# A linear recurrence with two dense layers on one core: transposes a slot sooner, a second tile for the inverse, x awaited in parts

## The reference, cut to what matters

```python
def _attn_ref(r, k, v, w, a, b):            # batch 4, heads 8, 768 tokens, head size 40
    for t in range(S):
        y[:, :, t] = einsum('bhd,bhde->bhe', rt, state)
        Sa = einsum('bhde,bhe->bhd', state, at)
        state_decay = state * wt[:, :, None, :] - einsum('bhd,bhe->bhde', Sa, bt)
        state = state_decay + einsum('bhd,bhe->bhde', vt, kt)
x = y as (3072 tokens, 320)
h = x @ w_in; g = maximum(0.01 * h, h); x = g @ w_out                    # 2048 wide
out = (1 / (1 + exp(-(x @ w_gate))) * (x @ w_val)) @ w_out2              # 1536 wide
```

## Time and profile before

| what | value |
|---|---|
| median of 3 runs | 1114.42 us (1110.23 to 1117.06) |
| profiled execution | 1112.1 us, span 1110.3 us |
| granted TensorE clock, mean | 0.972 |
| TensorE busy | 1046.9 us (94%), 16106 products and as many weight loads |
| VectorE busy | 617.0 us (56%) |
| ScalarE busy | 406.4 us (37%) |
| GpSimd busy | 142.9 us (13%) |
| idle of TensorE before products `a` (L642), ended by GpSimd | 23.3 us in 6 waits |

### The profile page before, as it was taken

One profiled execution on the slowest core, in us unless ns is written; L12 is line 12 of the kernel. 1 busy time (PEld: TensorE's weight loads), 2 busy tenths in 40 slices (PEclk: granted clock), 3 DMA queues, 4 the chain that ended last, 5 costly groups with the idle time before them and its releaser, 6 DMA issues.

```text
span 1110.3 us, 37363 instructions
## 1 busy us (share of the span) xinstructions
PE 1046.9 (94%) x16106; PEld 889.8 (80%) x16106; DVE 617.0 (56%) x2026; ACT 406.4 (37%) x830; POOL 142.9 (13%) x179
## 2 busy tenths in 40 slices
PE   2977979999998999999999999999999999999998
PEld 2866868787887877787887788888888888888887
DVE  7888898869687777776663244343232222323221
ACT  2243334345444443543443345432222232222222
POOL 6313130312213130303000000000000000000000
PEclk9987679999999999999999999999999999999999
DMA  5657254354425343533433043120202002020000
GB/s 173 174 171 187 60 131 95 89 111 108 112 63 134 87 112 64 153 81 73 105 90 63 9 149 115 62 85 1 62 1 63 1 3 59 1 62 1 24 1 24
DMA packets 133863, 87.68 MB, mean 79 GB/s; under 512 B 98274, under 2 KB 113634, under 8 KB 133700
## 3 DMA queue, kind: packets, MB, share of 16 engines
q1 hardware_dynamic: 126740, 62.85, 23.1%
q0 software_dynamic: 6960, 22.45, 6.8%
HBM read 66.39 MB, written 18.87 MB: 77 GB/s over the span
## 4 chain that ended last, share of the span: by engine, by line
PE 88%; issue 4%; DMA 3%; DVE 2%; POOL 2%; SPq 1%; ACT 1%; ACTq 0%; POOLq 0%; DVEq 0%
PE bank L824 17%; PE bank L874 12%; PE pair L874 12%; PE bank L839 4%; PE bank L840 4%; PE bank L841 4%; PE bank L894 4%; PE bank L892 4%; PE bank L893 4%; PE bank L910 2%; PE bank L799 2%; PE bank L843 2%; PE bank L844 2%; PE bank L786 2%; PE bank L642 2%
## 5 line engine op out<-in xcount | busy, mean ns | idle before, releaser
L1330 DVE TENSOR_TENSOR g_lo<-g_full,g_hi 128x512 fp32r<-128x512 f32 x168 | 120.7, 718 | 216.6 <-ACT g_hi L1082 216.4
L1082 ACT CAST g_hi<-g_full 128x512 fp32r<-128x512 f32 x168 | 104.4, 621 | 134.7 <-DVE g_full L1383 131.6
L824 PE MATMUL bank<-x_hi,w_up 128*128 128x512 f32 x480 | 136.6, 415 | 5.3 <-ACT x_hi L1092 3.2
L1278 DVE TENSOR_TENSOR prod<-t_unit,p_unit 128x31 f32<-128x31 f32 (+4 forms) x720 | 131.1, 222 | 5.4 <-ACT t_unit L1016 3.2
L1283 DVE TENSOR_TENSOR t_unit<-t_unit,prod 128x31 f32<-128x31 f32 (+4 forms) x720 | 132.8, 224 | 0.8
L1075 ACT ACTIVATE g_full<-bank 128x512 f32<-128x512 f32 x96 | 57.5, 599 | 188.7 <-PE bank L824 188.6
L824 PEld LDWEIGHTS bank<-x_hi,w_up 128*128 128x128 f32 x480 | 86.6, 192 | 24.8 <-ACT x_hi L1092 3.3
L1383 DVE TENSOR_TENSOR g_full<-pair,h_sb 128x512 f32<-128x512 f32 x36 | 24.9, 692 | 112.7 <-PE pair L874 112.0
L824 PE MATMUL bank<-x_lo,w_up 128*128 128x512 f32 x288 | 82.7, 396 | 0.0
L839 PE MATMUL bank<-g_hi,w_dn 128*128 128x512 f32 x192 | 77.5, 404 | 0.0
L1383 DVE TENSOR_TENSOR g_full<-bank,h_sb 128x512 f32<-128x512 f32 x36 | 24.9, 692 | 94.6 <-PE bank L874 86.3
(11 more groups left out here) (149 smaller groups left out, 2406.4 us busy)
## 6 DMA issues: line engine op xcount, KB each, us to landing
p_unit<-p_dram SPq DMA_DIRECT2D x48, 128.0 KB, 2.9
stage<-in_w_out POOLq DMA_DIRECT2D x7, 640.0 KB, 5.5
v_tok<-in_vT SPq DMA_DIRECT2D x12, 320.0 KB, 3.0
v_nu<-in_vN SPq DMA_DIRECT2D x24, 160.0 KB, 5.9
x<-y_sb SPq DMA_DIRECT2D x48, 80.0 KB
k_sb<-in_kF POOLq DMA_DIRECT2D x22, 160.0 KB, 3.6
v_sb<-in_vF SPq DMA_DIRECT2D x22, 160.0 KB
r_sb<-in_rF SPq DMA_DIRECT2D x22, 160.0 KB
```

Source lines behind the costliest of these rows:

```text
L824: last = nc.tensor.matmul(up_bank(m)[:], lhs, rhs, start=(e == 0), stop=(e == len(products) - 1))
L1082: nc.scalar.copy(g_hi[:, m % 2], g_full[:]).then_inc(g_hi_ready, 1)
L1278: nc.vector.tensor_tensor(terms, t_unit[:, e:m:2, t:t + 1].to_broadcast([P, rows, rest]), p_unit[:, t, t + 1:C].unsqueeze(1).to_broadcast( ...
L1330: nc.vector.tensor_tensor(g_lo[:, m % 2], g_full[:], g_hi[:, m % 2].bitcast(F32), ALU.subtract).then_inc(g_lo_ready, 1)
```

## The change

Seven edits. TensorE's `kb` and ScalarE's copies of them move from slot 7 to slot 6 of each window. `t_unit` gets a second half, taken in turn by units, and `act_t_unit` waits for the store of the unit before the last instead of the last; it stands in slot 7 of every window. `first` writes its eight columns into four, upper and lower partitions side by side, so that the copy to `u_first` is 160 wide instead of 320, and `p_cross` is half as large. The first up group of a block waits for each third of `x_hi` and `x_lo` ahead of the product that reads it. `act_out` waits for each of the four batches by a semaphore of its own. The fill entry ("sn", 0) goes from 56 to 40. `dve` reads and writes `t_unit[:, u % 2]` in all columns. The order of SyncE, GpSimd and VectorE is the same.

```diff
-        p_cross = sb(ctx, "p_cross", [P, 2, 2, TQ, C])
+        p_cross = sb(ctx, "p_cross", [P, 2, 2, TQ // 2, C])
...
-        t_unit = sb(ctx, "t_unit", [P, C // 2, C])
+        t_unit = sb(ctx, "t_unit", [P, 2, C // 2, C])
...
-                    sp.dma_start(dst[z], t_unit[z * MX:(z + 1) * MX]).then_inc(t_stored, 16)
+                    sp.dma_start(dst[z], t_unit[z * MX:(z + 1) * MX, u % 2]).then_inc(t_stored, 16)
...
-                    last = nc.tensor.matmul(o[first_rows(i, q), q * D:(q + 1) * D], t_sb[upper(i), c, q, 0:C],
+                    last = nc.tensor.matmul(o[first_rows(i, q), q % HQ * D:(q % HQ + 1) * D], t_sb[upper(i), c, q, 0:C],
                                             rhs_sb[upper(i), q], start=True, stop=True)
...
-                    last = nc.tensor.matmul(rhs_place(q)[lower(i)], p_cross[first_rows(i, q), u % 2, c, q],
-                                            u_first[first_rows(i, q), q], start=False, stop=True,
+                    last = nc.tensor.matmul(rhs_place(q)[lower(i)], p_cross[first_rows(i, q), u % 2, c, q % HQ],
+                                            u_first[first_rows(i, q), q % HQ], start=False, stop=True,
                                             skip_group_check=True)
...
             blk, f = divmod(m, NF1)
-            if f == 0:
-                pe.wait_ge(x_hi_ready, 3 * (blk + 1))
-                pe.wait_ge(x_lo_ready, 3 * (blk + 1))
...
             for e, (lhs, rhs) in enumerate(products):
+                if f == 0 and e < 3:
+                    pe.wait_ge(x_hi_ready, 3 * blk + e + 1)
+                elif f == 0 and e >= 5:
+                    pe.wait_ge(x_lo_ready, 3 * blk + e - 4)
                 last = nc.tensor.matmul(up_bank(m)[:], lhs, rhs, start=(e == 0), stop=(e == len(products) - 1))
...
                 last = nc.tensor.matmul(o, g_lo[:, par, tok], wt[:, 0, f % GT], start=False, stop=(f == NF2 - 1))
+                if f == NF2 - 1 and b < B - 1:
+                    last.then_inc(out_multiplied, 1)
             last.then_inc(down_multiplied, 1)
...
-        FILL = {("kb", -1): 2, ("sn", 0): 56,
+        FILL = {("kb", -1): 2, ("sn", 0): 40,
...
-                    elif s == 7 and soon:
+                    elif s == 6 and soon:
                         pe_kb(pe, n + 2)
                         pe_kb(pe, n + 3)
                         fill(pe, "kb", g)
...
-                    last = nc.scalar.mul(p_cross[first_rows(i, q), u % 2, c, q:q + HQ],
+                    last = nc.scalar.mul(p_cross[first_rows(i, q), u % 2, c],
                                          src[upper(i), q:q + HQ, C:L], -1.0)
...
-            wait(act, t_stored, 32 * u)
-            if u > 0:
-                columns_done(act, u - 1, C - 1)
-            nc.scalar.copy(t_unit[:].rearrange("p r t -> p (r t)"), restart[:, 1:2].to_broadcast([P, C // 2 * C])
+            wait(act, t_stored, 32 * (u - 1))
+            nc.scalar.copy(t_unit[:, u % 2].rearrange("p r t -> p (r t)"), restart[:, 1:2].to_broadcast([P, C // 2 * C])
                            ).then_inc(zeros_set, 1)
...
-            nc.scalar.copy(u_first[:], bank[bank_of("first", n)][:, 0:DM].rearrange("p (q d) -> p q d", d=D)
+            nc.scalar.copy(u_first[:, 0:HQ], bank[bank_of("first", n)][:, 0:HQ * D].rearrange("p (q d) -> p q d", d=D)
                            ).then_inc(bank_emptied[bank_of("first", n)], 1)
...
-            act.wait_ge(down_multiplied, M1 + NF2 * (blk + 1))
             act.wait_ge(o_stored, 48 * NJ)
             wait(act, o2_stored, 64 * blk)
             for b in range(B):
+                if b < B - 1:
+                    act.wait_ge(out_multiplied, (B - 1) * blk + b + 1)
+                else:
+                    act.wait_ge(down_multiplied, M1 + NF2 * (blk + 1))
                 nc.scalar.copy(o_tok(b), bank[DOWN2[b]][:, 0:DM]).then_inc(o2_evicted, 1)
...
                     elif s == 6 and soon:
                         act_sn(act, n + 2)
-                        if later and g >= 2:
-                            act_t_unit(act, g + 2)
-                    elif s == 7:
-                        if soon:
-                            act_kb(act, n + 2)
-                            act_kb(act, n + 3)
-                        if later and g < 2:
-                            act_t_unit(act, g + 2)
+                        act_kb(act, n + 2)
+                        act_kb(act, n + 3)
+                    elif s == 7 and later:
+                        act_t_unit(act, g + 2)
```

More of the change, by code:

```diff
@@ L190, in rwkv_mlp_kernel @@
         o_stored = sem("o_stored")
+        out_multiplied = sem("out_multiplied")
         o2_evicted = sem("o2_evicted")
@@ L1015, in act_t_unit @@
                 rows = slice(z * MX, (z + 1) * MX)
-                last = nc.scalar.copy(t_unit[rows].rearrange("p r t -> p (r t)")[:, z::C + 2],
+                last = nc.scalar.copy(t_unit[rows, u % 2].rearrange("p r t -> p (r t)")[:, z::C + 2],
                                       restart[rows, 0:1].to_broadcast([MX, C // 2]))
@@ L1277, in inverse_columns @@
                     wait(dve, column_ready[e], done[e])
-                    nc.vector.tensor_tensor(terms, t_unit[:, e:m:2, t:t + 1].to_broadcast([P, rows, rest]),
+                    nc.vector.tensor_tensor(terms, t_unit[:, u % 2, e:m:2, t:t + 1].to_broadcast([P, rows, rest]),
                                             p_unit[:, t, t + 1:C].unsqueeze(1).to_broadcast([P, rows, rest]), ALU.mult
@@ L1282, in inverse_columns @@
                     dve.wait_ge(column_multiplied[e], done[e] + 1)
-                    nc.vector.tensor_tensor(t_unit[:, e:m:2, t + 1:C], t_unit[:, e:m:2, t + 1:C], terms, ALU.add
+                    nc.vector.tensor_tensor(t_unit[:, u % 2, e:m:2, t + 1:C], t_unit[:, u % 2, e:m:2, t + 1:C], terms, ALU.add
                                             ).then_inc(column_ready[e], 1)
```

## The result

The changed kernel took 1141.78 us (median of 4 runs, 1138.70 to 1145.39) beside 1114.43 us (4 runs, 1110.23 to 1117.06) for the kernel before on the same chip: ratio 1.0274, 95% interval 1.0222 to 1.0326. I had forecast 1105.7, with 1 chance in 20 for slower by over 1%. The profiled run of the changed kernel took 1145.39 us and is the slowest of its four; that of the kernel before took 1112.1.

A forecast was written before the change was run, and what follows sets the result against it. TensorE was taken to set the pace from about 160 us, a recurrence's waits before; 1.6 + 1.5 + 3.1 + 1.2 + 1.3 = 8.7 us off the 1114.42 median gave 1105.7 us, range 1098 to 1113.

The forecast's parts named there:

- Transposes a slot sooner: Scan from window 2: k and b transposes 3.7 us sooner, winning 3.1 us of `a_sb` waits and 1.2 of clock.
- Now GpSimd will be through. By TensorE that is worth nothing: Block's `x_lo`: GpSimd's early finish ends the slow casts (4.49 against 1.90 us), worth nothing once x is awaited in parts.
- a stage where it waits for `g_hi` anyway: 0: From window 2, clearing in slot 7 starts VectorE's columns 0 to 6 some 0.5 us later, costing 0.
- My slower one: Early k and b fetch makes x late in five blocks by 3.7 us each, 18.5 lost; near 1124, chance 0.07.
- the unknown of 3 us: Idle times without releaser, some 9 us in eight places between 210 and 630 us, shift: 0, give or take 3.
- The waits for `a_sb` behind 160 us: TensorE's two waits for GpSimd's scaling, 0.81 us at 251.9 and 2.33 at 354.2, were to go: 3.1 us.
- At the fills: Start, fills 56 to 40: 3.6 us idle, clock 0.5, `st` sum at 62 to 63; 1.6 us won.
- Up(0): Block 0's first up group starts 2.0 us sooner with x awaited in parts; `g_lo` of step 0 leaves 0.3.
- start and block 0: Fewer fills were to win 1.6 us at the start, and x part by part 0.3 in block 0.
- The last issue of SyncE: Kernel's end: last copies and issues lie under products, last issue 0.5 us behind the last product; 1.3 us won.
- The second tile: Start: ScalarE's 12.42 us wait and VectorE's 3.25 us delay for the inverse tile go; counted 0, up to 1.0.
- the boundary of code: Start: the 4.07 us idle at 56.45 read as late code; 16 fewer fills move what follows 64 instructions against packets.

The follow-up runs named there:

- e3: Changed kernel with one more wait: from window 3 GpSimd fetches k and b only after slot 0's up group; 1116.15 us, ratio 1.0114.
- e9: Changed kernel with k and b still fetched early, but GpSimd scaling only once VectorE is through column 10; 1110.53 us, ratio 1.0002.
- e7: Changed kernel with the inverse's tile cleared in slot 6 again, from window 2 on; 1134.18 us, ratio 1.0165.
- e10: e9 with slot 0's `g_lo` ahead of columns 7 to 10 and the tile cleared in slot 6; 1110.57 us, ratio 0.9996.
- e12: Kernel before with only VectorE's order in slot 0 changed, `g_lo` ahead of columns 7 to 10; 1113.04 us, ratio 0.9990.
- e2: Kernel before with only the transposes and their copies a slot sooner, the one tile cleared behind them in slot 6; 1132.80 us, ratio 1.0234.
- e11: Changed kernel with slot 0's `g_lo` ahead of columns 7 to 10, the tile cleared in slot 6, no added GpSimd wait; 1110.18 us, ratio 1.0015.
- e5: Changed kernel with k and b fetched early, but GpSimd scaling only after slot 0's `rhs` products, from window 3; 1140.23 us, ratio 1.0220.
- e6: Changed kernel with GpSimd's scaling of a, b and k replaced by memsets from half n = 8 on; 1106.63 us, ratio 0.9976.

## Why the prediction was wrong

**The step that failed** is "Transposes a slot sooner": "GpSimd ... gains the 3.7 us", priced by who waits for GpSimd (`a_sb`, 3.1 us) and not by whom its scaling meets when it runs 3.7 us sooner. The needed rows were in the trace of before: the k scaling at 297.21 against `g_lo` at 296.21 leaves 1.0 us, so 3.7 us sooner must reach into the columns. What the runs showed in place of a gain of 3.1 us is eight waits for `g_lo` of slot 0, 29.0 us, and 13.3 us more of busy time in the scan. The same step also missed that the transposes had been TensorE's cover for this `g_lo`: 3.5 us of slack before, 0.9 left. Without GpSimd's early scaling this costs nearly nothing (2.0 us of waits in e3, 1.5 in e9); with it nearly the whole 4.98 us becomes a wait. I had the mechanism in hand, read from `x_lo` (4.49 against 1.90 us), and carried it only to the place where the collision ends: "Now GpSimd will be through. By TensorE that is worth nothing". It did end: `x_lo` is at 686 ns at the median and at most 693 in the changed kernel. The collision went to the columns, where e9 shows that it is worth some 30 us. The Trainium skill, SBUF — State Buffer, section Who interferes with whom, says that a VectorE instruction with two SBUF inputs and a GpSimd instruction that reads SBUF shut each other out. The columns have two SBUF inputs, and for VectorE the 4.98 us lost beside 4.84 us of four scalings agree with it; GpSimd's own scalings there hardly show it, with 1.18 to 1.28 us.

**The second size missed** is "a stage where it waits for `g_hi` anyway: 0" for the later clearing. It is true of the `g_lo` of slot 7 and not of the next one: with columns 0 to 10 in one stretch, VectorE had 0.9 us of slack at `g_lo` of slot 0 (257.13 against 257.99) in the changed kernel without the collision. e7 puts the place of the clearing at 8 to 12 us of the 27, from 4 runs each and over two batches, so roughly; of waits its trace has 3.9 us less. It costs only because the slack had been used up: in e9 it stands where the change has it, and e10, which moves it, gains nothing.

**The rivals.** My slower one had x late by the early fetch; in the changed kernel's trace TensorE waits 0.72 us for x at 150.39 and nowhere behind it. The right mechanism was none of them, and the range had to miss. The range had a fault of its own: its lower end takes in the unknown of 3 us, its upper end does not, and with it all bounds together would end near 1116.

**What came as forecast.** The waits for `a_sb` behind 160 us, 3.1 us, are gone, but they are back where the scaling is held back (4.1 us in six in e9). At the fills there are 3.69 us idle at 47.40 (3.6 forecast), four records in 1.15 us behind it, the short idle time inside `st` (1.37 at 60.03, in place of 4.07), and the `st` sum at 61.94 (62 to 63 forecast, 64.26 before). But 1.1 of these 2.3 us stood before the first of the fills (36.49 against 37.61), ahead of anything that the fills could have done, so 1.2 us are theirs and the rest is luck. Up(0) starts at 150.39, and `g_lo` of step 0 limits what is kept: 159.11 against 160.62. That is 1.5 us, beside the 1.9 that start and block 0 were to bring, and it is within the scatter: this `g_lo` stands at 154.49 in e12, which has the start of the kernel before, and at 154.8 to 160.9 in the eleven traces with the changed start. So no gain of the start is shown to reach the scan. The v transfer took a part of it (2.58 us at 155.57), which I had not named. The last issue of SyncE is at 1141.34; TensorE's last product ends near 1140.75, so the last issue comes 0.6 us behind it instead of 1.84: 1.25 won, 1.3 forecast. From the dense stage's first `x_lo` to the end of the span it is 401.9 us against 403.0 in the kernel before. The second tile took VectorE's idle time for `t_unit` in the start away and gave nothing, as said.

**Left open.** These terms, without the transposes, make some 3 to 4 us. e9 has them, and its interval leaves room for 4 us of gain at most; it does not show one. Start and scan differ by several us from run to run: the first `x_lo` came at 144.9 us in e12 and at 151.8 in the profile of before, with the same order of work up to there, and I did not find out why. Whether the boundary of code really moved, as I had read the 4.07 us, stays a reading. An idle time of 3.6 to 4.1 us without releaser ahead of `ut` is in all three traces with 56 fills (before, e2, e12) and in none of the eleven with 40, so it went with the changes to the start; but the eleven have the other edits of the start as well, and no run moved code alone.

## To carry to other kernels

Work that is let go sooner on an engine off the path still lands somewhere: before it is moved, read which instructions of the other engines will run beside it, and whether one of them stands ahead of something that is due. Here one wait on GpSimd, behind column 10, gave back some 30 us (e9), and so did putting what TensorE waits for ahead of the columns on VectorE, with the tile cleared earlier (e11). Work that is moved may also have been the cover of something: the transposes were that for `g_lo`, 3.5 us of slack before and 0.9 after. A wait that is to keep two engines apart has to be placed by the trace: with less than two columns still to run it was worth nothing (e5).

## What the runs showed of the hardware

- A pair of small VectorE column instructions (0.29 to 0.36 us) took 1.3 us beside one GpSimd scaling of 128x512, and 2.37 beside two in a row (e5, 252.37). GpSimd's scalings hardly lengthened: 1.18 to 1.28 us beside the columns in the changed kernel, at most 1.63 beside `g_lo` and `x_lo` (a scaling of `a_sb` in e9 and in the kernel before). Beside the columns VectorE loses about the whole of GpSimd's time, 4.98 us for 4.84.
- Memsets on GpSimd, which read nothing, cost the columns nothing (e6, 209 and 214 ns beside 249 and 251), nor does the issue of a fetch there. In the changed kernel the pair at 258.42 stays shut out over the issue of the a fetch and the scaling behind it, 2.28 us, and so does the one at 254.66 in e5; why the issue counts there and not in e6 is open.
- With eight idle times of TensorE of 1.1 to 4.2 us each, 29.0 us in all, its busy time in the scan rose by 13.3 us: the granted clock was 0.72 over the 6 us behind one of them and 1.00 in the next 6, and 0.96 in the mean against 0.99. The profiled run is the slowest of its four, so 13.3 us is at the high end.
